# Fused attention and two MLPs on one core: masks between two products, and weight halves made on VectorE

## The reference

```python
# q, k, v, a_re, a_im: (batch 4, heads 8, seq 768, head_dim 48)
mag = sqrt(a_re**2 + a_im**2); scale = minimum(mag, 0.999) / (mag + 1e-6)
ar, ai = a_re * scale, a_im * scale
for t in range(768):                       # S_re, S_im: (4, 8, 48, 48)
    S_re, S_im = ar[t] * S_re - ai[t] * S_im + outer(k[t], v[t]), ar[t] * S_im + ai[t] * S_re
    y[t] = einsum('bhd,bhde->bhe', q[t], S_re)
x = y as (3072 tokens, 384)
h = x @ w_in;  x = (h * clip(h + 3, 0, 6) / 6) @ w_out                          # 384 -> 2048 -> 384
h = x @ w2_in; x = (maximum(h, 0) + alpha * minimum(h, 0)) @ w2_out             # 384 -> 2048 -> 384
```

## Time and profile before

| | |
|---|---|
| runs | 1044.53, 1047.25, 1047.72 us; median 1047.25 |
| profiled execution | 1048.43 us, span 1046.7 us |
| TensorE busy | 964.3 us (92%), mean granted clock 0.983 |
| VectorE busy | 613.1 us (59%) |
| ScalarE busy | 491.2 us (47%) |
| GpSimd busy | 308.7 us (29%) |

### The profile page before, as it was taken

One profiled execution on the slowest core, in us unless ns is written; L12 is line 12 of the kernel. 1 busy time (PEld: TensorE's weight loads), 2 busy tenths in 40 slices (PEclk: granted clock), 3 DMA queues, 4 the chain that ended last, 5 costly groups with the idle time before them and its releaser, 6 DMA issues.

```text
span 1046.7 us, 17244 instructions
## 1 busy us (share of the span) xinstructions
PE 964.3 (92%) x6594; PEld 871.1 (83%) x6594; DVE 613.1 (59%) x1066; ACT 491.2 (47%) x881; POOL 308.7 (29%) x275
## 2 busy tenths in 40 slices
PE   0787799789999999999999999999999999999997
PEld 0676799789999999999999998888888888888886
DVE  6857877767887878778874244453343333434332
ACT  7666677666667766667663354221121111211211
POOL 2076222112222222222222233233232322333232
PEclk9988999889999999999999999999999999999999
DMA  8532333333433233333321251001010010100000
GB/s 245 159 102 57 82 84 85 81 75 84 97 91 93 69 92 79 77 97 98 71 76 39 100 196 53 1 1 61 0 61 1 1 61 1 35 27 0 31 1 31
DMA packets 80931, 70.50 MB, mean 67 GB/s; under 512 B 32592, under 2 KB 78160, under 8 KB 80464
## 3 DMA queue, kind: packets, MB, share of 16 engines
q1 hardware_dynamic: 80208, 68.80, 24.1%
q10 hardware_dynamic: 640, 0.59, 0.2%
HBM read 40.90 MB, written 9.44 MB: 48 GB/s over the span
## 4 chain that ended last, share of the span: by engine, by line
PE 70%; DVE 18%; issue 6%; ACT 4%; SPq 1%; DMA 0%; POOL 0%; DVEq 0%; ACTq 0%
PE op L1173 10%; PE hp L1174 10%; PE hp L1173 10%; PE op L1174 10%; PE hp L1175 10%; PE op L1175 10%; PE yp L1161 4%; PE gp L1168 3%; DVE t_fb L834 3%; DVE scores L856 2%; DVE t_fb L840 2%; DVE t_phase L806 2%; DVE gated L885 2%; ACT gate L617 2%; DVE prod L849 1%
## 5 line engine op out<-in xcount | busy, mean ns | idle before, releaser
L517 POOL TENSOR_TENSOR g_lo<-gated,g_hi 128x384 fp32r<-128x384 f32 (+2 forms) x240 | 271.9, 1133 | 683.1 <-ACT g_hi L624 683.1
L624 ACT ACTIVATE g_hi<-gated 128x384 fp32r<-128x384 f32 (+2 forms) x240 | 129.9, 541 | 357.4 <-DVE gated L900 284.4
L896 DVE TENSOR_SCALAR gate<-hp,alpha_sb 128x512 f32<-128x512 f32 x96 | 72.1, 751 | 240.0 <-PE hp L1175 240.0
L1173 PE MATMUL op<-g_hi,wb_hi 128*128 128x384 f32 (+1 forms) x432 | 144.2, 334 | 4.9 <-POOL wb_lo L523 3.3
L1173 PE MATMUL hp<-x_hi,wa_hi 128*128 128x384 f32 (+1 forms) x432 | 142.0, 329 | 4.7 <-DVE gated L885 3.4
L885 DVE SCALAR_TENSOR_TENSOR gated<-gate,hp 128x384 f32<-128x384 f32 (+1 forms) x144 | 72.7, 505 | 125.7 <-ACT gate L617 125.3
L1175 PE MATMUL hp<-x_hi,wa_lo 128*128 128x384 f32 (+1 forms) x432 | 138.9, 322 | 0.0
L1174 PE MATMUL hp<-x_lo,wa_hi 128*128 128x384 f32 (+1 forms) x432 | 138.9, 321 | 0.0
L1174 PE MATMUL op<-g_lo,wb_hi 128*128 128x384 f32 (+1 forms) x432 | 138.7, 321 | 0.0
L1175 PE MATMUL op<-g_hi,wb_lo 128*128 128x384 f32 (+1 forms) x432 | 138.7, 321 | 0.0
L617 ACT ACTIVATE gate<-hp,half 128x384 f32<-128x384 f32 (+1 forms) x144 | 77.1, 535 | 94.0 <-PE hp L1175 93.9
(11 more groups left out here) (107 smaller groups left out, 1635.3 us busy)
## 6 DMA issues: line engine op xcount, KB each, us to landing
st<-prod SPq DMA_DIRECT2D x92, 145.1 KB, 2.9
a_sb<-a_in SPq DMA_DIRECT2D x24, 288.0 KB, 4.0
qk_sb<-qk_in SPq DMA_DIRECT2D x24, 288.0 KB, 3.7
v_pad<-v_in SPq DMA_DIRECT2D x24, 192.0 KB, 3.8
x_raw<-x SPq DMA_DIRECT2D x6, 768.0 KB, 5.7
out<-out_sb SPq DMA_DIRECT2D x6, 768.0 KB, 3.9
st<-prod SPq DMA_DIRECT2D x96, 32.2 KB, 2.2
wa_raw<-w_in SPq DMA_DIRECT2D x6, 512.0 KB, 7.8
```

Of the source, the lines that this page charges most:

```text
L517: pool.tensor_tensor(g_lo[:, at, 0:wide], gated[:, at * UT:at * UT + wide], g_hi[:, at, 0:wide].bitcast(F32), ALU.subtract).then_inc(glo_d ...
L624: act.activation(g_hi[:, at, 0:wide], gated[:, at * UT:at * UT + wide], ACT.Copy).then_inc(ghi_done, 1)
L896: dve.tensor_scalar(gate[:, at], hp[:, n % 2, 0:wide], 0.0, alpha_sb[:, m:m + 1], ALU.min, ALU.mult).then_inc(gate_done, 1)
L1173: pe.matmul(acc, lhs[0], rhs[0], start=start, stop=False)
```

## The change

It has three parts. First, at step C `product(c1, 0)` stands ahead of the two masks of c0 and `product(c1, 1)` behind them; before, both products stood ahead of them. In slots of 7 or 8 items the products move from item 1 to item 2 as well. Second, the low halves of the first MLP's weights are made on VectorE instead of GpSimd: eight blocks in pairs at four places ahead of the first items, the others at the end of the items. Third, `ALONE` is 2 instead of 4: the slots of chunks 2 and 3 begin two items earlier and have 6 and 7 items, and `STEPS` has an entry for 7. Along with these, ScalarE does `angle(3)` ahead of `high(2)` and not behind it, and VectorE does `gate1(1)` ahead of `state(1)`.

```diff
-STEPS = {5: (0, 1, 1, 2, 3, 3, 4), 6: (0, 1, 1, 2, 3, 3, 4), 8: (0, 1, 2, 3, 4, 5, 6)}
+STEPS = {5: (0, 1, 1, 2, 3, 3, 4), 6: (0, 1, 1, 2, 3, 3, 4), 7: (0, 1, 1, 2, 3, 4, 5),
+         8: (0, 1, 2, 3, 4, 5, 6)}
-ALONE = 4
+ALONE = 2
 # gpsimd: split_w is gone
-            for w in range(W_EARLY):
-                split_w(w)
-            for k in range(GSTEP):
-                low(k)
-            for n in range(NT - GSTEP):
-                low(n + GSTEP)
-                for w in splits_at(n):
-                    split_w(w)
+            for n in range(NT):
+                low(n)
 # scalar
             for n in range(ALONE):
                 gate_of(n + GSTEP)
-                high(n + GSTEP)
                 if n == 0:
                     angle(3)
+                high(n + GSTEP)
 # vector: product(c, x) has the three waits and one of the two products
+            def split_w(n):
+                lo, landed, hi, at = w_part(n)
+                dve.wait_ge(w_hi_done, n + 1)
+                dve.tensor_tensor(lo[:, at], landed[:, at], hi[:, at].bitcast(F32), ALU.subtract
+                                  ).then_inc(w_lo_done, 1)
             state(0)
+            split_some(2)
             mask(1, 0)
             mags(3)
             forward(2)
             mask(1, 1)
             backward(2)
+            split_some(2)
             x_low(1)
             products(2)
             gate1(0)
+            split_some(2)
+            gate1(1)
             state(1)
-            gate1(1)
             decay_parts(3)
             gate1(2)
             mags(4)
-            for n in range(1, ALONE):
-                gate1(n + GSTEP)
+            split_some(2)
+            for n in range(ALONE):
+                if n > 0:
+                    gate1(n + GSTEP)
+                for w in splits_at(n):
+                    split_w(w)
 # vector, in the slots
                 if "B" in steps and c1 is not None:
                     backward(c1)
-                    products(c1)
                 if "C" in steps:
+                    if c1 is not None:
+                        product(c1, 0)
                     mask(c0, 0)
                     mask(c0, 1)
+                    if c1 is not None:
+                        product(c1, 1)
 ...
                     if c3 is not None:
                         mags(c3)
+                for w in splits_at(n):
+                    split_w(w)
```

More of the change, by code:

```diff
@@ L518, in low @@
                                    g_hi[:, at, 0:wide].bitcast(F32), ALU.subtract).then_inc(glo_done, 1)
[L520 to L524, removed]
             pool.memset(v_pad[:, :], 0.0).then_inc(pads_set, 1)
@@ L840, in backward, with product @@
                 dve.tensor_tensor(every(t_fb), every(t_fb), every(qk_sb), ALU.mult).then_inc(qb_done, 1)
-            def products(c):
+            def product(c, x):
                 dve.wait_ge(trig_set, c + 1)
@@ L847, in products @@
                 dve.wait_ge(qb_done, c + 1)
[L848 to L851, removed]
+                dve.tensor_tensor(prod[:, x, :, :, 0:CH].rearrange("p k q t -> p q k t"), t_fb[:, :, :, :],
+                                  t_trig[:, x, :, :].unsqueeze(1).to_broadcast([P, 2, KT_DM, CH]), ALU.mult
+                                  ).then_inc(prod_done, 1)
+            def products(c):
+                product(c, 0)
+                product(c, 1)
+            def split_w(n):
[3 more added lines that the diff above has]
+                                  ).then_inc(w_lo_done, 1)
             def mask(c, k):
@@ L927, in _, with split_some @@
             dve.wait_ge(consts_set, 2)
+            splits = iter(range(W_EARLY))
+            def split_some(count):
+                for _ in range(count):
+                    split_w(next(splits))
             def decay_parts(c):
```

## The result

The changed kernel takes 1021.63 us (median of 4 runs, 1017.19 to 1022.83), the kernel before 1047.49 us: a ratio of 0.975, 95% interval 0.9714 to 0.9786. The forecast was 1017.9 us in a range of 1009 to 1031.

The account below looks back on a forecast made before the run. TensorE, busy 964.3 of 1046.7 us, bounds the kernel, so gains come from its idle or slow time. Terms 2.5 + 7.7 + 4.2 + 2.0 + 12.9 = 29.3 us off 1047.25 give 1017.9 us, range 1009 to 1031.

Parts of the forecast that it names:

- The masks: In every slot, with the second product behind them, the masks end 1.5 us earlier, limited to 1.4 on 256 columns.
- the long stretch: Slots on 384 columns, 235 to 600 us: TensorE's waits for the masks nearly vanish, 12.9 us gained.
- The rival of a new wait: Long stretch: TensorE waits for `gate1` or `low` instead, giving back 6.5 us: 1024.4 us, chance 0.13.
- Chunks 6 to 8: Slots of chunks 6, 7 and 8: 4.2 us from a shorter VectorE chain and 2 us from TensorE's clock.
- the chain: Slots of chunks 6 to 8: the path through VectorE sets the pace and shortens, 4.2 us over three slots.
- the clock: Slots of chunks 6 to 8: shorter waits let TensorE run less slowly, 2 us, between 0 and 5.
- the landing of the copies: Chunk 7's slot: the last six DMAs land 0.3 us before TensorE needs them, capping one of three slots.
- The start: Before the first items: VectorE instructions no longer stretched by GpSimd's splits, 2.5 us gained, bounds 1.4 and 2.5.
- The first slots: Slots of chunks 2 and 3: earlier phases and unstretched VectorE instructions, less the splits' cost, gain 7.7 us, bounds 4 and 12.
- The price of the splits: First items and slots: a split takes 0.69 us on VectorE; 12 splits in the slot cost 7.3 us.
- the signs named ahead: Profile after: mask waits gone, chunk 2's outputs at some 78 us, 3 to 4 us wait ahead of first `output`.
- The slower case: Items 0 to 7: VectorE and ScalarE wait for each other and lose their overlap: 1054 us, chance 0.04.

Follow-up runs that it names:

- masks_only: Kernel before with the second product moved behind the masks and nothing else: 1020.88 us, ratio 0.9733.
- masks_undone: Changed kernel with both products ahead of the masks again: 1042.55 us, ratio 0.9945.
- splits_only: Changed kernel with four items alone and both products ahead of the masks again, so only the splits are moved to VectorE: 1043.98 us, ratio 0.9971.
- alone_only: Kernel before with two items instead of four ahead of the slots, splits still on GpSimd, products ahead of the masks: 1046.45 us, ratio 0.9985.
- early_pair: Changed kernel with VectorE's splits of blocks 7 and 8 between gate1(1) and state(1) instead of behind mags(4): 1018.41 us, ratio 0.9713.
- two_copies_on_act: Changed kernel with the two big sine copies of chunks 7 and 8 issued by ScalarE's queue beside SyncE's: 1019.57 us, ratio 0.9723.
- loads_later: Changed kernel with four weight loads (three of w_in, one of w_out) issued behind the copies of chunk 0's products: 1022.60 us, ratio 0.9754.

## Why the prediction was right, and where its terms were off

**The masks** were the right place and the right mechanism. masks_only, with nothing else, reaches a ratio of 0.9733, and masks_undone, with all the rest, 0.9945. The second product did cost the masks about 1.5 us, because a `low` ran beside it: in the changed kernel a product never takes longer than 0.962 us, and the masks keep 0.68 us beside a `low`. By the Trainium skill, SBUF — State Buffer, section "Who interferes with whom", a VectorE instruction with two SBUF inputs contends with a GpSimd one that reads SBUF, and one with at most one SBUF input, outside the two-port modes, does not; the trace agrees with this for products and masks. The term for the long stretch was 12.9 us; it measured 14.1. The 14 waits of 13.16 us went entirely, the one of 1.76 too, of which 0.3 were expected to stay; the other 0.9 us are busy time of TensorE. The rival of a new wait there did not come about: 368.68 of 368.68 us are busy.

**Chunks 6 to 8** were put at 4.2 us for the chain and 2 for the clock, 6.2 together; they gave 6.9, in masks_only 7.4. The same slots before, for the second line of the first rows above:

```profile
174.12:243.73 69.61, 59.80 (x567) 0.88 0.36 88
```

In the same 567 instructions TensorE's busy time fell by 4.3 us, while the clock rose from 0.88 to 0.95, and its idle time fell from 9.8 to 7.2 us, by 2.6. So the waits gave less than their 4.2 us and the busy time more than the 2 of the clock's term: the sum came out near by luck. This is a count and not a separation of causes, since TensorE's slower matmuls are a link of the chain as well. The waits for the masks fell to 1.54, 0.85 and 0.86 us, not to the 2 us I expected, since the landing of the copies came in between, as the text feared: 1.60 us ahead of chunk 7's scores and 2.33 us ahead of chunk 8's. The prediction let this cap one of the three slots; it capped two.

**The start** is the step that failed. Its 2.5 us took it that the end of VectorE's work decides when the copies land. In splits_only the copies are issued 1.9 us earlier and TensorE begins at the same 31.23 us; with four weight loads out of their way it begins at 28.6 to 29.0 us in three kernels, earlier than in any of the eleven others. So the weight loads beside the copies decide their landing, and an earlier issue was worth nothing for it. The changed kernel's profile has the first item 1.7 us later than before, and the first scores 2.3 us later. In masks_only, whose start is the start of before, they are 1.2 and 2.1 us later, so a difference of this kind comes without any edit there. What is left of the term is the 0.6 us that splits_only shows at equal first scores. Taken as 0.6 instead of 2.5, the sum would be 27.4 us and 1019.9 us, against 1021.63 and 1019.53 measured.

**The first slots** were put at 7.7 us and gave 6.5. In single parts, from the first item to chunk 4's first wait, masks_only saves 2.4, splits_only 4.1 and alone_only 1.2 us, 7.7 together; all parts at once save 6.6. These are single profiles. The first `output` waited 4.19 us, forecast 3.5. Its successor in early_pair shows that this wait was not the bound: VectorE's chain was. The phases of chunk 3 began 16.8 us behind the first item instead of 20.4, 3.5 us sooner, where 4.6 were forecast; the splits of items 0 and 1 wait for ScalarE for 1.27 us there, and later in the slots three wait for 1.56, 1.00 and 1.01 us, more than the 0.4 us an item that I had as a bound. The price of the splits themselves held: 0.71 and 0.74 us in the mean, with 0.69 forecast. Of the signs named ahead, chunk 2's outputs were to begin at some 78 us and began at 84.05; 4.2 us of that are the start. VectorE's phases take 1.22 us in the first slots, but 1.66 for chunk 5 and up to 2.00 later, about as before.

**The slower case** did not come about: TensorE's only waits for a `low` are 0.80 and 0.17 us, in the slots of chunks 4 and 5, which have no splits. Splits and lows do stretch each other, as the slower rival feared: the `low` at 59.28 us takes 1.25 instead of 0.73 us, and the split at 66.33 us, beside a `low`, 1.21 instead of 0.68. TensorE's 4.19 us ahead of the first `output` contain this half microsecond.

## What to carry to other kernels

When two consumers wait for one engine, ask which of its instructions each consumer needs, and in what order they can be interleaved: here one product before the masks and one behind them is worth 2.0 to 2.7%, both behind lose about two fifths of that to the copies, both in front lose all. Before counting a stage that ends earlier as a gain, look at what its result is queued behind: here copies beside a bulk load landed no earlier for an earlier issue. Where moving one thing away only brings other waits of nearly the same length, as in two_copies_on_act, two chains are balanced; an edit would have to shorten both, which no run here tried.

## What the runs showed of the hardware that was not expected

With the weight loads in the same place the start differs between executions: first scores at 30.73 to 33.55 us in eleven profiles. The share of time in which the DMA engines are busy differs along with it. In the profile with 31.23 us before, it was 0.48 from 26 to 32 us; in the changed kernel's, with 33.55 us, 1.05 (the profile's share can pass 1), while they moved 168 instead of 128 GB/s. In the four profiles with first scores at 30.73 to 31.30 us the share is 0.48 to 0.74, in the seven from 32.44 us on 0.77 to 1.05. In part this only says that late copies are still on their way then. The load of `wb_raw` took 11.7 us to land in the one and 14.2 in the other, a small copy of `st` 2.4 and 6.9 us. Whether the small copies slow the loads, or only wait for them, stays open. In loads_later, where fewer of them meet in the first 36 us, the loads of `wa_raw` land after 6.0 instead of 8.4 us and the smallest copies after 2.5 us.
